# Extra work placed inside the waits of a two-engine pipeline, one search step fewer, a shorter first search: a gated-memory layer with routed experts on one Trainium2 core

## What is computed

```python
x = ...                                  # (3072, 320) out of the memory layer
logits = x @ w_gate                      # (3072, 8)
order = np.argsort(-logits.flatten())    # tokens are dealt greedily, best logit first
for idx in order:
    tok, e = (int(idx) // E, int(idx) % E)
    if assigned[tok] >= 0 or counts[e] >= cap:
        continue
    assigned[tok] = e
    counts[e] += 1
for e in range(E):
    mask = assigned == e
    h = np.maximum(x[mask] @ w1[e], 0.0)         # 320 -> 1024
    out[mask] = h @ w2[e]                        # 1024 -> 320
h = out @ w_in                                   # 320 -> 2048
g = np.maximum(h, 0.0) + alpha * np.minimum(h, 0.0)
return g @ w_out                                 # 2048 -> 320
```

## Time and profile before

| | |
|---|---|
| median of 3 runs | 849.48 us (846.57 to 853.49) |
| the profiled execution, its own time | 847.56 us |
| its span (first to last instruction) | 845.5 us |
| PE busy | 768.7 us (91%) |
| DVE busy | 586.9 us (69%) |
| ACT busy | 321.6 us (38%) |
| POOL busy | 164.2 us (19%) |
| mean granted clock of TensorE | 0.956 of full speed |

### The profile page before, as it was taken

How to read it: one execution, slowest core, us unless ns; L and a number is a source line. 1 busy time by engine, 2 the same in 40 slices (tenths; PEclk the granted TensorE clock), 3 DMA queues, 4 the chain that set the end, 5 groups by cost and what they waited for, 6 DMA issues and landing times.

```text
span 845.5 us, 16938 instructions
## 1 busy us (share of the span) xinstructions
PE 768.7 (91%) x5446; PEld 713.1 (84%) x5446; DVE 586.9 (69%) x1503; ACT 321.6 (38%) x775; POOL 164.2 (19%) x245
## 2 busy tenths in 40 slices
PE   4999999952399999999999999999999999999995
PEld 3999999941288988998898889889988988998995
DVE  5767777765757786777678677867777786775342
ACT  4656666500313432351344134323513441352331
POOL 7367777400100120011001101100110021011001
PEclk9999999955599999999999999999999999999998
DMA  6788888300500410230040005003100400040000
GB/s 156 197 232 217 242 221 216 91 29 1 165 1 1 148 34 9 75 91 23 0 136 28 23 0 164 23 0 112 52 23 0 136 28 23 30 135 24 1 1 23
DMA packets 73406, 65.76 MB, mean 78 GB/s; under 512 B 35232, under 2 KB 64544, under 8 KB 73376
## 3 DMA queue, kind: packets, MB, share of 16 engines
q1 hardware_dynamic: 63584, 51.94, 22.2%
q0 software_dynamic: 2688, 8.65, 3.2%
q10 hardware_dynamic: 7104, 4.79, 1.8%
HBM read 56.71 MB, written 8.65 MB: 77 GB/s over the span
## 4 chain that ended last, share of the span: by engine, by line
PE 56%; DVE 25%; issue 10%; ACT 6%; DMA 1%; DVEq 0%; POOL 0%; SPq 0%; ACTq 0%; POOLq 0%
PE bank L805 11%; PE bank L807 9%; PE bank L806 8%; DVE g_act L1436 7%; ACT h_hi L1041 5%; PE bank L665 5%; PE bank L712 5%; PE bank L823 3%; PE bank L824 2%; PE bank L700 2%; PE bank L693 2%; PE bank L746 2%; PE bank L676 2%; DVE by_row L1371 2%; DVE w_lo L1409 1%
## 5 line engine op out<-in xcount | busy, mean ns | idle before, releaser
L1041 ACT CAST h_hi<-g_act 128x384 fp32r<-128x384 f32 x128 | 65.8, 514 | 175.8 <-DVE g_act L1436 175.8
L805 PE MATMUL bank<-wo_hi,h_hi 128*128 128x320 f32 x384 | 121.4, 316 | 0.6 <-DVE h_lo L1441 0.6
L807 PE MATMUL bank<-wo_hi,h_lo 128*128 128x320 f32 x384 | 118.6, 309 | 0.0
L806 PE MATMUL bank<-wo_lo,h_hi 128*128 128x320 f32 x384 | 118.0, 307 | 0.0
L1441 DVE TENSOR_TENSOR h_lo<-g_act,h_hi 128x384 fp32r<-128x384 f32 x128 | 71.5, 558 | 59.9 <-ACT h_hi L1041 58.0
L589 POOL DMA_INDIRECT xe<-x_rows,idx_in x24 | 23.4, 974 | 445.1 <-DVE idx_in L1379 388.4
L1037 ACT ACTIVATE h_hi<-bank 128x384 fp32r<-128x384 f32 x64 | 31.5, 492 | 163.4 <-PE bank L824 163.4
L805 PE MATMUL bank<-yT_hi,wi_hi 128*128 128x384 f32 x256 | 93.1, 364 | 0.3 <-DVE yT_lo L1462 0.3
L1436 DVE SCALAR_TENSOR_TENSOR g_act<-g_neg,rest_alpha,bank 128x384 f32<-128x384 f32 x128 | 78.2, 611 | 20.1 <-ACT g_neg L1039 18.3
L807 PE MATMUL bank<-yT_hi,wi_lo 128*128 128x384 f32 x256 | 86.6, 338 | 0.0
L806 PE MATMUL bank<-yT_lo,wi_hi 128*128 128x384 f32 x256 | 86.6, 338 | 0.0
(11 more groups left out here) (218 smaller groups left out, 1802.9 us busy)
## 6 DMA issues: line engine op xcount, KB each, us to landing
s<-w SPq DMA_DIRECT2D x8, 1280.0 KB, 9.3
s<-w SPq DMA_DIRECT2D x8, 1024.0 KB, 5.3
s<-w SPq DMA_DIRECT2D x16, 256.0 KB, 6.3
k_in<-kT SPq DMA_DIRECT2D x24, 160.0 KB
q_wide<-qT SPq DMA_DIRECT2D x48, 80.0 KB
k_row<-k SPq DMA_DIRECT2D x24, 160.0 KB, 3.2
v_in<-v SPq DMA_DIRECT2D x24, 160.0 KB, 3.8
gate_o<-o SPq DMA_DIRECT2D x24, 160.0 KB, 2.7
```

The source lines that it names most:

```text
L805: pe.matmul(acc, ah, bh, start=start, stop=False, skip_group_check=True)
L806: pe.matmul(acc, ah, bl, start=False, stop=False, skip_group_check=True)
L807: return pe.matmul(acc, al, bh, start=False, stop=stop, skip_group_check=True)
L1041: act.copy(h_hi[:, k % 3, :], g_act[:, k % 3, :]).then_inc(g_hi, 1)
```

## The change

- **Search steps.** Nine steps in place of ten, eight of them with 31 trial values and one with 15; before there were four with 31 and six with 15. The router's keys are cut accordingly (value bits 24 and not 23, tie bits 8 and not 9; not shown).
- **First round.** `first_compare` writes the comparison in two halves of 12 columns; `first_count` counts each column with a matmul of its own (24 of 31x8) and starts on the first half while DVE writes the second. `own_blocks`, `add_four` and the reduction in `flag_full` are gone there. Rounds within experts keep their form.
- **First rows.** Each of the three gathers of the first expert has its own semaphore, and `turn_first` transposes a block when it has landed.
- **Blocks inside waits.** On ACT `high_w1` and `high_w2` stand between `g_neg` and `h_hi`. On DVE `take`, `close`, `place_members`, `match_rows`, `reopen`, `choose_tie`, `low_in` and `low_out` stand between `g_act` and `h_lo`. With one step fewer, everything behind the search moves one tile forward, the transposes of the next rows too (behind tiles 11 to 13, not 12 to 14). `read_tokens` waits no longer for `rows_in`.
- **Gate maximum.** `neg_peak` is made by a scalar_tensor_tensor with a row of -1.0 (`minus_row`, a new memset) as second tensor, in place of a tensor_scalar.
- **End.** The last expert has no round to carry; of its last three tiles, the sums of tiles 13 and 14 now come first for all three blocks, and tile 15 is last.

```diff
-    VALUE_STEPS = [(5, 18), (5, 13), (5, 8), (4, 4), (4, 0)]
-    TIE_STEPS = [(5, 19), (4, 15), (4, 11), (4, 7), (4, 3)]
+    VALUE_STEPS = [(5, 19), (5, 14), (5, 9), (5, 4), (4, 0)]
+    TIE_STEPS = [(5, 18), (5, 13), (5, 8), (5, 3)]
...
-                                            bass.IndirectOffsetOnAxis(ap=idx_in[:, t:t + 1], axis=0)).then_inc(rows_in, 16)
+                                            bass.IndirectOffsetOnAxis(ap=idx_in[:, t:t + 1], axis=0)).then_inc(first_rows[t] if first(e, 1) else rows_in, 16)
...
+            def first_count(n):
+                for half in range(2):
+                    pe.wait_ge(halves_ready, 2 * n + half + 1)
+                    for c in range(NT // 2 * half, NT // 2 * half + NT // 2):
+                        ins = pe.matmul(CNT[0:JM, 0:E], above[:, JM * c:JM * c + JM], choice[:, c, :],
+                                        start=(c == 0), stop=(c == NT - 1), skip_group_check=True)
+                ins.then_inc(count_ready, 1)
...
+            pe.sem_inc(four_ready, NS)
             for n in range(NS):
-                count(0, n)
-                add_four(0, n)
+                first_count(n)
+            def turn_first():
+                for m in range(CT):
+                    pe.wait_ge(first_rows[m], 16)
+                    for t in range(3):
+                        ins = pe.transpose(ACC[t][:, m * P:m * P + P], xe[:, m, t * P:t * P + P], ident[:, :])
+                        if m == CT - 1:
+                            ins.then_inc(xe_turned, 1)
-                    pe.wait_ge(rows_in, 16 * CT * (e + 1))
-                elif not first(e, 1):
+                    pe.wait_ge(rows_in, 16 * CT * e)
+                else:
-                row = ACC[t] if first(e, 1) else ROW
-                    ins = pe.transpose(row[:, m * P:m * P + P], xe[:, m, t * P:t * P + P], ident[:, :])
+                    ins = pe.transpose(ROW[:, m * P:m * P + P], xe[:, m, t * P:t * P + P], ident[:, :])
...
-                           between=(ph, J1 + j - 1) if route and j < 3 else None)
+                           between=(ph, J1 + j - 1) if route and j < 2 else None)
-                    if route and j < 3:
+                    if route and j < 2:
-                    if route and j == 4:
+                    if route and j == 3:
                         rank_members(ph)
-                    if route and j < 2:
+                    if route and j < 1:
                         count(ph, J1 + j)
-                    if route and j == 2:
+                    if route and j == 1:
                         count_taken(ph)
-                    if route and j == 8:
+                    if route and j == 7:
                         list_tokens(ph)
-                    if more and 12 <= j < 15:
-                        turn_rows(e + 1, j - 12)
+                    if more and 11 <= j < 14:
+                        turn_rows(e + 1, j - 11)
-                    down2(J2 - 3, (0, 1))
-                    down2(J2 - 2, (0, 1))
-                    down2(J2 - 1, (0, 1))
-                    for j in range(J2 - 3, J2):
+                    for j in range(J2 - 3, J2 - 1):
+                        down2(j, (0, 1))
+                    for j in range(J2 - 3, J2 - 1):
-
-            for t in range(3):
-                turn_rows(0, t)
+                    down2(J2 - 1)
+
+            turn_first()
...
+                    if meanwhile:
+                        meanwhile[0](*meanwhile[1:])
-                    activate(e, k)
+                    j = k - J1
+                    block = None
+                    if more and 9 <= j < 12:
+                        block = (high_w1, e + 1, j - 9)
+                    if more and 12 <= j < 15:
+                        block = (high_w2, e + 1, j - 12)
+                    activate(e, k, block)
-                    j = k - J1
-                    if more and 9 <= j < 12:
-                        high_w1(e + 1, j - 9)
-                    if more and 14 <= j:
-                        rows_hi(e + 1, j - 14)
-                    if more and 12 <= j < 15:
-                        high_w2(e + 1, j - 12)
+                    if more and 13 <= j:
+                        rows_hi(e + 1, j - 13)
-                    rows_hi(e + 1, 2)
...
-                dve.tensor_scalar(neg_peak[0:n, g, :], peak[0:n, g, :], carry[0:n, g:g + 1], -1.0, ALU.max, ALU.mult).then_inc(gate_logs, 1)
+                dve.scalar_tensor_tensor(out=neg_peak[0:n, g, :], in0=peak[0:n, g, :], scalar=carry[0:n, g:g + 1],
+                                         in1=minus_row[0:n, :], op0=ALU.max, op1=ALU.mult).then_inc(gate_logs, 1)
...
+            def first_compare(n):
+                J = 2 ** STEPS[n][0] - 1
+                tie = n >= len(VALUE_STEPS)
+                key = key2 if tie else best_value
+                base = TIE_BASE if tie else VALUE_BASE
+                if n not in (0, len(VALUE_STEPS)):
+                    dve.wait_ge(base_ready, n)
+                for half in range(2):
+                    cs = slice(NT // 2 * half, NT // 2 * half + NT // 2)
+                    st = steps[:, n, 0:J].unsqueeze(1).to_broadcast([P, NT // 2, J])
+                    if n in (0, len(VALUE_STEPS)):
+                        dve.tensor_tensor(above_chunks(J)[:, cs, :], bc(key[:, cs], J), st, ALU.is_ge).then_inc(halves_ready, 1)
+                    else:
+                        dve.scalar_tensor_tensor(out=above_chunks(J)[:, cs, :], in0=bc(key[:, cs], J), scalar=base,
+                                                 in1=st, op0=ALU.subtract, op1=ALU.is_ge).then_inc(halves_ready, 1)
+            def first_flag(ch, n):
+                J = 2 ** STEPS[n][0] - 1
+                dve.wait_ge(count_ready, n + 1)
+                ch.link(dve.tensor_tensor(hit[0:J, :], CNT[0:J, 0:E], need[0:J, :], ALU.is_ge))
+                dve.tensor_reduce(flag[0:J, :], hit[0:J, :], X, ALU.max).then_inc(flag_ready, 1)
...
-                if not first(ph, 1):
-                    dve.wait_ge(rows_in, 16 * CT * ph)
...
-                compare(ch, 0, n)
-                own_blocks(ch, 0, n)
-                flag_full(ch, 0, n)
+                first_compare(n)
+                first_flag(ch, n)
+            dve.sem_inc(blocks_ready, NS)
+            dve.sem_inc(above_ready, NS)
+            dve.sem_inc(dve_step, NS)
+            ch.n += NS
...
-                    if route and j < 2:
+                    if route and j < 1:
                         own_blocks(ch, ph, J1 + j)
+                    if route and j == 8:
+                        read_tokens(ch, ph)
+                    block = None
+                    if route and j == 0:
+                        block = (take, ch, ph)
+                    if route and j == 2:
+                        block = (close, ch, ph)
-                        close(ch, ph)
-                    if route and j == 9:
-                        read_tokens(ch, ph)
+                        block = (place_members, ch, ph)
+                    if route and 4 <= j < 7:
+                        block = (match_rows, ch, ph, j - 4)
+                    if route and j == 7:
+                        block = (reopen, ch)
+                    if route and j == 8:
+                        block = (choose_tie, ch, slice(0, NT))
+                    if more and 9 <= j < 12:
+                        block = (low_in, e + 1, j - 9)
+                    if more and 12 <= j < 14:
+                        block = (low_out, e + 1, j - 12)
-                        split_hidden(e, J1 + j + 2, ((compare, ch, ph, J1 + 1) if j == 0 else (take, ch, ph)) if route and j < 2 else None)
-                    if route and j == 4:
-                        place_members(ch, ph)
-                    if route and 5 <= j < 8:
-                        match_rows(ch, ph, j - 5)
-                    if route and j == 8:
-                        reopen(ch)
+                        split_hidden(e, J1 + j + 2, block)
+                    if route and j == 7:
-                    if route and j == 9:
-                        choose_tie(ch, slice(0, NT))
-                    if more and 10 <= j < 13:
-                        low_in(e + 1, j - 10)
-                    if more and 12 <= j < 15:
-                        rows_lo(e + 1, j - 12)
-                    if more and 13 <= j < 15:
-                        low_out(e + 1, j - 13)
+                    if more and 11 <= j < 14:
+                        rows_lo(e + 1, j - 11)
```

More of the change, by code:

```diff
@@ L225, in build_program @@
         ones_row = ga("ones_row", [P, P])
+        minus_row = ga("minus_row", [P, P])
         cum_f = ga("cum_f", [P, 2, P])
@@ L293, in build_program @@
         above_ready = sem("above_ready")
+        halves_ready = sem("halves_ready")
         count_ready = sem("count_ready")
@@ L317, in build_program @@
         rows_in = sem("rows_in")
+        first_rows = [sem(f"first_rows{t}") for t in range(CT)]
         xe_turned = sem("xe_turned")
@@ L1030, in rows_hi, with activate @@
```

(9 more changed lines are left out.)

## The result

The changed kernel takes 825.94 us in the median of 4 runs (821.14 to 826.35), the kernel before 849.46 in 4 runs on the same chip: a ratio of 0.9715, 95% interval 0.9686 to 0.9745. 830.6 (824.5 to 840) was forecast. The profiled execution takes 826.35 us, its span 824.6, which is 20.9 under the span before.

A forecast was written before the change was run, and what follows sets the result against it. PE was taken as the bound nearly everywhere but the first routing round. Start 0.3, first round 4.6, experts 14.0 and end 0 sum to 18.9 us off the 849.48 median: 830.6 us, eight in ten from 824.5 to 840.

The forecast's parts named there:

- the end gave nothing: Last expert's final tiles: the new order of sums was taken to gain nothing, bounds -0.6 and +0.4 us.
- The parts forecast at 18.6 us: First round and seven experts together: -4.6 us and -14.0 us.
- -2.0 was forecast: Each of seven experts with a round: 2.0 us less, bounds -0.5 and -2.4, -14.0 us in all.
- The waits for `xT_lo` go: -1.6 per expert: Last tiles of each expert: PE's transposes no longer wait for DVE's `xT_lo`, 1.6 us less.
- The -0.2 for the list of tokens: Each expert: PE's wait for `by_row` goes because DVE's comparisons end earlier, 0.2 us less.
- The 3.22 us after which PE was to ask: Experts' last tiles: PE asks for `xT_lo` after 3.22 us, while it needs about 2.1 from its transposes.
- DVE is now quicker than PE: Experts' last tiles: with weights inside the wait, DVE's tile takes 2.2 us, 2.7 with `xT_lo`, against PE's 2.73 bare.
- First round: -4.6 forecast: First routing round: 26.09 us becomes 21.5, with 31-value steps of 2.37 us and the 15-value step 1.97.
- The count was the unknown: First round: cost of a 31-column weight load with 8-column matmul, bounds 0.03 and 0.13 us; count-bound above 0.044.
- Rows of the first expert: nothing forecast: Between first round and first expert: earlier transposes gain nothing, up to 0.5 us in either direction.
- Start: 0.3 forecast: Gate maximum: the hold behind POOL's memsets moves from `neg_peak` to the next cast, gaining 0.3 us, bounds 0 and 3.6.
- The clock: a rival: First expert's start: full clock granted earlier or later, 2 us either way, 828.6 or 832.6 us; chance 8%.

The follow-up runs named there:

- blocks_out: The changed kernel with ACT's and DVE's weight blocks behind each tile again, routing blocks still inside waits, transposes still early: 823.28 us, experts 74.02 us.
- after_again: The changed kernel once more, unaltered, measured beside the other runs: 822.16 us, ratio 0.9690.
- round_old: The changed kernel with the first round's old comparison, four-column counts, blocks and their sum, still nine steps: 825.91 us, first round 25.28 us.
- rank_late: The changed kernel with `rank_members` called behind `down(3)` instead of ahead of it: 822.11 us, experts 73.54 us.
- all_out: The changed kernel with weight and routing blocks behind their tiles, none inside a wait but `take`, transposes still early: 836.23 us, experts 75.78 us.
- late_rows: The changed kernel with the next rows' transposes and their splitting one tile later again, blocks still inside waits: 829.23 us, experts 74.78 us.
- late_out: The changed kernel with weight blocks behind tiles and transposes one tile later, routing blocks still inside waits: 831.37 us, experts 74.91 us.

## Why the prediction was right

- **Right in kind and sign.** DVE got ahead of PE and the waits for `xT_lo` went, the end gave nothing, the cast took over the hold.
- **The total: within the range in part by luck.** The parts forecast at 18.6 us gave 25.7. Taken off 849.46 that is 823.8, just under the 824.5 of the range; the 825.94 inside it goes with more half clock in the memory layer than before, which no term of the forecast has. Of the four runs, the three with a mean granted clock of 0.952 or 0.953 took 825.65 to 826.35, and the one with 0.958 took 821.14.
- **Experts: a size was off.** -2.0 was forecast, -2.88 came. The term is "The waits for `xT_lo` go: -1.6 per expert": it took the listed waits for the lost time, and the stretch measured 2.41. The -0.2 for the list of tokens is too small for the same reason, 0.36 from start to start. With -0.5 for the step, +0.24 for the rank and +0.09 for the sum behind the eighth ReLU tile (327.95 to 331.17 after, 331.62 to 334.75 before) this is -2.94. The two terms are 1.0 us in each of seven experts, most of what the parts gave beyond the forecast. The 3.22 us after which PE was to ask is too long likewise: it asks after 3.06, and the room for `xT_lo` was 0.7 us and not 1.1.
- **Experts: the reason was half right.** "DVE is now quicker than PE" holds, but the 1.22 us of weights inside the wait aren't what decides it. A tile of 2.8 us against 2.73 was measured so in `blocks_out`, and by itself it makes 0.18 us of wait; the lag brought along from the tiles of routing, and the transposes' place, make the rest. The prediction gave neither a term. That the weights inside would have sufficed without the routing inside is possible, and no run tests it.
- **First round: -4.6 forecast, -5.16 measured.** A step of 31 values is 2.33 and not 2.37 (the 0.03 for reading PSUM didn't show: `hit` took 0.15 as before), which makes 0.3 in eight. The step of 15 values took 1.93 and not 1.97, and 0.2 lies in what I had carried over as 0.59 for the tie keys less the quicker first comparison: the two steps that begin so took 2.19 and 2.20, and the tie keys 0.65, so it is 0.38. The count was the unknown: 0.042 us a pair lies near the lower bound (0.03), and only just under the 0.044 from which a step would be count-bound.
- **Rows of the first expert: nothing forecast, -0.49 measured.** The transfer of the first weights took 9.79 us in this execution, 0.49 less than the earlier trace rows; that is all of it. It is scatter: the stretch takes from 19.28 (`after_again`, transfer 9.35) to 20.62 us (`round_old`, transfer 10.67) in kernels that are the same in it.
- **Start: 0.3 forecast, 0.07 measured.** The other parts behind the cast take 0.37 and 0.39 us in place of 0.23 and 0.29. The Trainium skill (page "SBUF — State Buffer", section "SBUF: two separate sides") held for which of them is held and which is not. By it the edit alone only moves the hold, and with the casts exchanged the hold is gone, an estimate of 3.6 us (the 3.87 of the earlier trace rows less 0.29); the traces show 0.05 and 3.4.
- **The clock: a rival that came at another place and larger.** I had 2 us at the end of the first round, and those didn't come: the granted clock is 0.50 past the start of the first expert (to 232 us), before and after. A change of the clock came in the memory layer. Windows of before and then of after, 40 to 50 and 60 to 70 us (PE's busy time is the second number; last three columns: granted clock, DMA share, GB/s):

```profile
40.00:50.00 10.00, 10.00 (x76) 9.41 (x76) 5.14 (x17) 3.63 (x13) 3.35 (x5) 0.83 0.89 223
...
60.00:70.00 10.00, 10.00 (x92) 9.77 (x92) 6.76 (x16) 5.85 (x22) 7.49 (x12) 1.00 0.79 206
```

```profile
40.00:50.00 10.00, 10.00 (x59) 9.18 (x58) 4.44 (x15) 3.11 (x11) 3.35 (x5) 0.67 0.92 227
...
60.00:70.00 10.00, 10.00 (x74) 9.50 (x73) 6.87 (x15) 6.85 (x25) 7.15 (x10) 0.83 0.76 204
```

PE is busy throughout, and yet goes at 1.2 GHz for part of these stretches, longer after than before. From 12 us to the first comparison the mean clock is 0.93 in the changed kernel (188.08) and in `after_again` (186.84), 0.95 in `rank_late` (186.00), in `all_out` (184.52) and before (183.25), all with PE's first L660 at 11.7 to 11.8. So the stage moves by 3.6 us between kernels that are the same in it. What remains between 183.25 and 184.5 or 186.0, and whether the change has a share in it, stays open: there is one trace of the kernel before. In the medians it is small: from 849.46 and 848.39 less 25.7 come 823.8 and 822.7, measured were 825.94 and 822.16. Beside `after_again`, at the same mean clock, it is small too: at 0.953 the kernel before took 848.95 and 850.18 and the changed one 824.87, at 0.958 they took 847.30 and 821.97 to 822.30, which is 24.1 to 25.3 us less each time.

## What to carry to other kernels

A list of waits that goes by modelled ends of matmuls shows too little: count from one start to the next, across the whole stretch. Where two engines hand work to each other, ask which lag one of them brings into the stretch, before blaming the work in it. When an operation is held behind another engine, exchange the whole row of its kind or none; one alone only moves the hold to its neighbour.

## What the runs showed of the hardware

- **The held cast is let in at some boundaries and not at others.** In three of the nine profiled executions that have both casts behind the new `neg_peak` (`round_old`, `blocks_out`, `late_rows`) each cast waited only for the memset that ran. DVE in `round_old`:

```profile
6.64 0.44 DVE L1126 CAST peak_parts<-neg_peak 128x128 bf16<-128x128 f32 x1
...
7.44 1.46 DVE L1129 CAST peak_parts<-neg_a 128x128 bf16<-128x128 f32 x1
```

The memset of `q_wide` ended there at 7.00 and that of `q_in` at 8.83, and the casts ended at 7.08 and 8.90. PE's L660 then starts at 9.62. In the other six the cast ended at 10.16 to 10.18, between the short memsets: in five of them both these boundaries passed, and in `late_out`, where it started at 7.05, just behind the first, the second and the end of `state`. Start times don't tell the two apart (6.56, 6.64 and 6.72 against 6.58 to 7.05). What decides it stays open. With the exchanged casts this draw is gone as well.
- **31-column weight loads with 8-column matmuls** go at 0.042 us a pair (1.00 / 24) at a granted clock of 0.50, no slower for each than the eight small ones of `list_tokens` at the same clock (0.37 / 8).
